# A scan, an MLP and routed experts on one core: the coupled steps written out in full, the first two in one list with the opening, and part of the q and k moves on a second queue

## The chip, the cores and the metric

The kernel runs on one core of a Trainium2 chip. The metric is the device time of one execution in microseconds (us), median of three. A core has TensorE (PE in the profile; PEld is its weight loads), VectorE (DVE), ScalarE (ACT), GpSimd (POOL) and SyncE (SP), which here does nothing but issue DMAs. Each engine runs its own list of instructions in order and waits on semaphores.

## What is computed

```python
for t in range(768):                 # 4 batches x 8 heads, head size 48, complex gates a
    S_re, S_im = a_re*S_re - a_im*S_im + k_t v_t, a_re*S_im + a_im*S_re
    y[t] = q_t . S_re                # a is first scaled so that |a| <= 0.999
x  = y as (3072 tokens, 384)
h  = x @ w_in                        # 384 -> 2048
x2 = (max(h,0) + alpha*min(h,0)) @ w_out      # 2048 -> 384
keep = x2 @ w_skip > 0; e = argmax(x2 @ w_gate)          # 8 experts
out = x2 + keep * p_e * relu(x2 @ w1[e]) @ w2[e]
```

## The kernel before

Phase 1 goes over 8 halves of 384 tokens (`HT`), each of three chunks of 128 tokens (`c` is 0, 1, 2). For a half, the scan part does: norms of the gates (`square_gates` to `norm_gates`), their running products within and across the chunk (`multiply_within`, `multiply_across`, `carry`; VectorE), the inverse of the products' size (`sum_products` to `inverse`), k scaled by it (`scale_k`), and q and k times the products (`decay`, once for the real part r=0, once for the imaginary part r=1). `move_qk` then brings each part with 5 DMAs from 128 rows of channels into `kq`, in which each head's real and imaginary rows stand together; `kq` is one buffer, so the moves of a chunk wait until the chunk before has been read. On TensorE a chunk is `turn_k` twice, `scores` twice, `values`, `carried_values` (what the state of the chunks before gives) and `outer`; VectorE masks the scores (`mask_scores`), ScalarE copies k back (`back_k`) and y out (`high_y`), VectorE takes y's low part (`low_y`), and `move_y` brings y with 6 DMAs into `xT`. The state goes `outer`, `add_state`, `scale_state` (ScalarE), `next_state`, `move_state` (4 DMAs), `carried_values` of the next chunk.

The MLP of a half is 16 times `up` (9 matmuls of 384 columns; float32 as high and low parts) and `down` (9 of 394 columns). Between them ScalarE does `bend_h` and `high_g`, VectorE `join_g` and `low_g`. `up(f)` needs `join_g(f-2)`, since `mlp_ps` has two banks.

The halves are coupled: a step works at once on the attention of half h, the MLP of half h-1 and the gates of half h+1. Its lists, one for each engine, are written out by hand in `step`. Steps 1 to 6 are a hardware loop of three rounds with two steps each; step 7 (no gates left) and the last half's MLP stand behind it. Ahead of it `first_step` is the opening: it does half 0's scan and attention, half 1's gates, and makes the MLP's weights. For these `load_turned(f)` and `load_whole(f)` (f is 0 to 15) bring rows of w_out, `gate_columns(f)` (TensorE) and `take_columns(f)` (ScalarE) add nine gate columns to them, `high_pack(f)` (ScalarE) and `low_pack(f)` (VectorE) split them; `split_w_in` and `low_w_in` do the same for w_in in six pieces. TensorE starts on step 1 when all of these are made:

```python
            first_step()
            pe.wait_ge(wi_lo, len(WI_PIECES))
            pe.wait_ge(wo_lo, NF)
            with pe.Fori(0, 3) as i:
                step(Half(i, 1), True)
                step(Half(i, 2), True)
```

All DMAs of phase 1 are issued by SyncE, one after the other, in the order of its own list.

Phase 2 sorts tokens by expert. A chain of small VectorE operations gives each token a slot (`slot_of`) and a row in it (`row_of`). Then in three groups of 8 token tiles VectorE makes `in_slot` (is_equal), `in_row` (is_equal, 128x1024) and `entries` (four columns a slot), and TensorE multiplies them to a table that says which token stands where. The table's first column is what the first gather waits for; behind the gather stand the experts' matmuls, bound by TensorE.

Of the kernel before, what the change touches and what calls it, by code (L numbers as in the profile page):

```python
# [13 lines left out]
P = 128  # L14
# [5 lines left out]
NC = 3  # L20
# [41 lines left out]
LAG = 3  # L62

# [74 lines left out]
def phase1(nc, qk, v, a, mask_in, w_in, w_pack, alpha, w_skip, w_gate, w1, w2, out, x2_rows,  # L138
           mlp_ps, out_ps, att_ps, ident, logits, arena, rows, x2_stored, first_loaded):
    with ExitStack() as ctx:  # L140
# [41 lines left out]
        g_parts = sb("g_parts", [P, 4, 2, HT], F32R)  # L182
        x2 = rows[:, 0:NC * DL].rearrange("p (i d) -> p i d", i=NC)
# [50 lines left out]
        qk_moved = sem("qk_moved")  # L234
# [39 lines left out]

        def filled_by(name, at_chunk):
            return filled(at_chunk[0], name, at_chunk[1])
# [20 lines left out]
        def _(sp):  # L297
            chunk_at = sp.alloc_register("chunk_at")
            half_at = sp.alloc_register("half_at")
            made_at = sp.alloc_register("made_at")  # L300
            used_at = sp.alloc_register("used_at")
# [34 lines left out]
            def move_qk(h, c, r):  # L336

                made = val(chunk_no(h, c) * 2 + (r + 1))
                if r == 0 and not back(h, c):
                    sp.wait_ge(zeroed, 5)  # L340
                if r == 0 and back(h, c):
                    bank, used = filled_by("y", back(h, c))
                    if not isinstance(made, int):
                        sp.reg_mov(made_at, made)
                        sp.reg_mov(used_at, used)
                        made, used = made_at, used_at
                    sp.wait_ge(bank, used)
                sp.wait_ge(qk_made, made)
                for p0, n, t0, nt, row, slot in OP_MOVES:
                    sp.dma_start(kq[UP * r + row:UP * r + row + n, slot:slot + nt, :, :],  # L350
                                 qk_dec[p0:p0 + n, r, t0:t0 + nt, :, :]).then_inc(qk_moved, 16)

            def move_factors(h):
                if not h.plus(-1).exists():
                    sp.wait_ge(zeroed, 5)
# [5 lines left out]
            def move_y(h, c):  # L361

                sp.wait_ge(*emptied(h, "y", c))
                for p0, n, t0, nt, row, pair in PAIR_MOVES:
# [22 lines left out]
            def step(h, mlp_too, more, ahead):  # L387
                n, nxt = h.plus(-1), h.plus(1)

                load_qkv(h, 1)  # L390
                move_qk(h, 1, 0)
                move_qk(h, 1, 1)
                load_qkv(h, 2)
                move_state(h, 0)
                move_y(h, 0)
# [9 lines left out]
                move_state(h, 2)  # L405
# [3 lines left out]
                if mlp_too:  # L409
                    store_x2(n)  # L410

# [31 lines left out]
            def first_step():  # L443
                first, second, third = Half(0, 0), Half(0, 1), Half(0, 2)
# [3 lines left out]
                load_small()  # L448
                load_gates(first, 2)
                load_turned(0)  # L450
                load_whole(0)
                load_turned(1)
                load_mask()
                load_whole(1)
# [1850 lines left out]
```

## Time and profile before

| | |
|---|---|
| three runs, median | 862.19 us (858.65 to 862.41) |
| the profiled execution | 858.82 us, its span 857.1 us |
| PE busy | 719.2 us (84%) |
| DVE busy | 610.4 us (71%) |
| ACT busy | 480.6 us (56%) |
| opening, to the first `up` | 0 to 125.4 us |
| steps 1 to 6 | 125.4 to 558.8 us |
| step 7, then the last MLP | to 626.3, then to 677.2 us |
| routing table, to the first gather | 677.2 to 700.7 us |
| gather and experts | to 857.1 us |

A matmul of 384 columns is shown with 0.34 us, but successive ones start 0.17 to 0.18 us apart; where the busy time of a stretch is used, overlaps count once. Start times in us are counted from the start of the span.

### The profile page before, as it was taken

The page shows a single profiled execution, that of the slowest core. Times are in us where ns is not written, and L with a number is a line of the kernel's source. Part 1 is how long each engine was busy: PE and PEld are TensorE (multiplying, and loading weights), DVE is VectorE, ACT ScalarE, POOL GpSimd, SP SyncE. Part 2 cuts the span into 40 slices and gives each one's busy share as a digit, 9 for nine tenths or more (in the row PEclk, how much of TensorE's full clock was granted, in tenths as well). Part 3 has the DMA queues.
Part 4 walks back from the last instruction along what each step waited for, and adds up shares of the span by engine and source line. Part 5 has one row for each costly group of instructions (what it writes and reads, how often), then busy time and mean ns, then how long its engine had stood idle before and what let it go on. Part 6 is the DMA issues. An engine that isn't in the chain of part 4 may idle for free. (4 is left out here: it accounts for less than half of the span.)

```text
span 857.1 us, 16221 instructions
## 1 busy us (share of the span) xinstructions
PE 719.2 (84%) x5454; PEld 695.8 (81%) x5454; DVE 610.4 (71%) x1252; ACT 480.6 (56%) x932; POOL 53.0 (6%) x57
## 2 busy tenths in 40 slices
PE   3334449998998999899899999999999639899996
PEld 3234349998998999889799898999999629899896
DVE  4996978997996898899699889964423373344443
ACT  7479169369649847936964993753432313233330
POOL 1000000000000000000000000000000113222222
PEclk9999679999999999999999999999999859899999
DMA  7643444344343433533533343244510276814200
GB/s 234 221 126 88 119 125 101 92 119 137 106 131 94 130 73 117 154 92 109 148 91 107 102 152 78 60 144 119 184 58 1 94 266 245 303 60 170 95 26 20
DMA packets 82443, 104.80 MB, mean 122 GB/s; under 512 B 15991, under 2 KB 68385, under 8 KB 82337
## 3 DMA queue, kind: packets, MB, share of 16 engines
q1 hardware_dynamic: 80544, 99.69, 38.9%
q0 software_dynamic: 1792, 3.76, 1.4%
q8 instruction: 59, 0.97, 0.5%
q14 instruction: 48, 0.39, 0.1%
HBM read 61.04 MB, written 12.19 MB: 85 GB/s over the span
## 5 line engine op out<-in xcount | busy, mean ns | idle before, releaser
L616 PE MATMUL mlp_ps<-xT,w_in_hi 128*128 128x384 f32 x768 | 203.1, 346 | 24.3 <-DVE g L1316 14.6
L626 PE MATMUL out_ps<-w_out_hi,g_parts 128*128 128x394 f32 x768 | 215.6, 346 | 0.0
L616 PEld LDWEIGHTS mlp_ps<-xT,w_in_hi 128*128 128x128 f32 x768 | 137.7, 190 | 32.6 <-DVE g L1316 21.4
L626 PEld LDWEIGHTS out_ps<-w_out_hi,g_parts 128*128 128x128 f32 x768 | 141.7, 188 | 0.8
L626 PE MATMUL out_ps<-w_out_lo,g_parts 128*128 128x394 f32 x384 | 131.0, 341 | 0.0
L616 PE MATMUL mlp_ps<-xT,w_in_lo 128*128 128x384 f32 x384 | 130.3, 339 | 0.0
L861 ACT ACTIVATE bent<-mlp_ps,bend_size 128x384 f32<-128x384 f32 x128 | 73.6, 575 | 90.7 <-PE mlp_ps L616 90.6
L1316 DVE SCALAR_TENSOR_TENSOR g<-mlp_ps,slope_side,bent 128x384 f32<-128x384 f32 x128 | 78.1, 611 | 57.7 <-ACT bent L861 57.4
L867 ACT ACTIVATE g_parts<-g 128x384 fp32r<-128x384 f32 x128 | 65.5, 518 | 39.4 <-DVE g L1316 35.4
L1321 DVE TENSOR_TENSOR g_parts<-g,g_parts 128x384 fp32r<-128x384 f32 x128 | 70.2, 550 | 14.5 <-ACT g_parts L867 14.4
L1982 ACT ACTIVATE hT<-mlp_ps 128x256 fp32r<-128x256 f32 x52 | 20.0, 384 | 98.6 <-PE mlp_ps L1918 98.6
L616 PEld LDWEIGHTS mlp_ps<-xT,w_in_lo 128*128 128x128 f32 x384 | 72.8, 190 | 0.0
L626 PEld LDWEIGHTS out_ps<-w_out_lo,g_parts 128*128 128x128 f32 x384 | 72.3, 188 | 0.0
L1918 PE MATMUL mlp_ps<-xT_e,w_sb 128*128 128x128 f32 x480 | 58.4, 284 | 8.0 <-issue 8.0
L1918 PEld LDWEIGHTS mlp_ps<-xT_e,w_sb 128*128 128x128 f32 x480 | 57.4, 199 | 9.5 <-issue 9.5
L2136 DVE SCALAR_TENSOR_TENSOR hT<-mlp_ps,hT 128x256 fp32r<-128x256 f32 x52 | 22.1, 424 | 60.1 <-ACT hT L1982 60.1
L855 ACT ACTIVATE s_t<-s_in,f_pair 112x96 f32<-112x96 f32 x192 | 55.0, 365 | 5.2 <-DVE s_in L1300 4.2
L1932 PE MATMUL out_ps<-w_hi,hT 128*128 128x384 f32 x208 | 56.6, 343 | 0.0
L703 PE MATMUL mlp_ps<-wgs,g 128*128 128x10 f32 x96 | 22.2, 367 | 38.0 <-DMA g<-in_w_pack 38.0
L551 PE MATMUL att_ps<-kq 112*128 112x128 f32 x384 | 52.9, 288 | 0.0
L703 PEld LDWEIGHTS mlp_ps<-wgs,g 128*128 128x128 f32 x96 | 21.4, 328 | 38.7 <-DMA g<-in_w_pack 28.1
L551 PEld LDWEIGHTS att_ps<-kq 112*128 112x128 f32 x384 | 50.5, 205 | 0.0
(157 smaller groups left out, 1208.0 us busy)
## 6 DMA issues: line engine op xcount, KB each, us to landing
kq<-qk_dec SPq DMA_DIRECT2D x96, 144.0 KB, 3.0
arena<-in_a SPq DMA_DIRECT2D x24, 384.0 KB, 4.2
arena<-in_qk SPq DMA_DIRECT2D x24, 384.0 KB, 4.7
w_sb<-in_w SPq DMA_DIRECT2D x6, 1536.0 KB, 7.5
w_raw<-in_w SPq DMA_DIRECT2D x6, 1536.0 KB, 12.2
xT<-y_parts SPq DMA_DIRECT2D x48, 144.0 KB, 2.7
arena<-in_w SPq DMA_DIRECT2D x4, 1536.0 KB, 9.2
v_nat<-in_v SPq DMA_DIRECT2D x24, 192.0 KB, 4.6
```

The costliest lines, as they stand in the source:

```text
L551: last = pe.matmul(ps[:, n * CH:(n + 1) * CH], kq[:, slot, 1, :], kq[:, slot, 0, :], start=True, stop=True)
L616: last = pe.matmul(ps[:, 0:HT], w_in_v[s][:, kk, f * P:(f + 1) * P], xT[n.p][:, kk, m, :], start=(kk == 0 and j == 0), stop=(kk == KT - 1 ...
L626: last = pe.matmul(out_ps[i][:, 0:DL], g_parts[:, f % 4, s, i * P:(i + 1) * P], w_out_v[m][:, f, :], start=(f == 0 and j == 0), stop=(f == ...
L703: last = pe.matmul(mlp_ps[f % 2][:, 0:GATE_COLS], turned_stage[f % DEPTH][:, kk * P:(kk + 1) * P], wgs[:, kk, :], start=(kk == 0), stop=(k ...
L855: last = act.activation(s_t[:, r, :, pair_, :], s_in[:, :, pair_, :], ACT.Copy, scale=f_pair[:, h.p, pair_, c, r:r + 1])
L861: act.activation(bent[:, f % 2, :], mlp_ps[f % 2][:, 0:HT], ACT.Relu, scale=bend_size[:, f:f + 1]).then_inc(bent_made, 1)
L867: act.activation(g_parts[:, f % 4, 0, :], g[:, f % 3, :], ACT.Copy).then_inc(g_hi, 1)
L1316: dve.scalar_tensor_tensor(out=g[:, f % 3, :], in0=mlp_ps[f % 2][:, 0:HT], scalar=slope_side[:, f:f + 1], in1=bent[:, f % 2, :], op0=ALU.m ...
L1321: dve.tensor_tensor(g_parts[:, f % 4, 1, :], g[:, f % 3, :], g_parts[:, f % 4, 0, :].bitcast(F32), ALU.subtract).then_inc(g_lo, 1)
L1918: last = pe.matmul(mlp_ps[g % 2][:, (f % 2) * P:(f % 2 + 1) * P], w1_v[p][:, kk, f * P:(f + 1) * P], xT[:, kk, :], start=(kk == 0), stop=( ...
L1932: last = pe.matmul(out_ps[0][:, 0:DM], hT[:, a, f, :], w2_v[p][b][:, f, :], start=(f == 0 and j == 0), stop=(f == NFE - 1 and j == 2))
L2136: dve.scalar_tensor_tensor(out=hT[:, 1, 2 * g:2 * g + 2, :].rearrange("p f t -> p (f t)"), in0=mlp_ps[g % 2][:, 0:2 * P], scalar=0.0, in1= ...
```

## The change

1. The loop is gone: steps 2 to 6 are written out one after the other, step 1 stands in one list with the opening (`first_steps`), and step 7 follows as before.
2. In `first_steps` only `low_pack(0)` to `(4)` stand ahead of the first `decay` on VectorE (before: 0 to 13), and `high_pack` and `low_pack` 13 to 15 stand among step 1's work. `up` and `down` of half 0 wait for their own weights.
3. Chunk 1 of half 0 has a second buffer for moved q and k, `kq_too`, which lies in `g_parts`, free until the first `high_g`. The two parts count on semaphores of their own, so `decay(r)` waits for the moves of its own part only.
4. Of half 0's moves, those of the imaginary parts (5 DMAs a chunk) and half of `move_y` for chunk 2 (3 DMAs) are issued by ScalarE, 18 in all.
5. The order within a step is new on every engine.
6. In phase 2 the table has three columns a slot for four, and 34 slots for 33; `in_row` of the third group is made by ScalarE, with eight Abs of 128x128 and one Relu of 128x1024; one small VectorE operation behind the table goes. ScalarE's `split(0)` stands behind that.

```diff
+        kq_too = g_parts[0:ROWS, :, :, :].rearrange("p a b t -> p (a b t)")[:, 0:HEADS * 2 * CH].bitcast(F32).rearrange(
+            "p (h w s) -> p h w s", h=HEADS, w=2)
...
+        def in_kq_too(h, c):
+            return val(h.n) == 0 and c == 1
...
+            def move_qk(h, c, r):
+                last_in = last_user_of_kq(h, c)
+                if last_in:
+                    act.wait_ge(*filled_by("y", last_in))
+                else:
+                    act.wait_ge(zeroed, 6)
+                act.wait_ge(qk_made, val(chunk_no(h, c) * 2 + (r + 1)))
+                for p0, n, t0, nt, row, slot in OP_MOVES:
+                    act.dma_start(kq_of(h, c)[UP * r + row:UP * r + row + n, slot:slot + nt, :, :],
+                                 qk_dec[p0:p0 + n, r, t0:t0 + nt, :, :]).then_inc(qk_moved[r], 16)
...
                     up(n, 3)
-                    up(n, 4)
                 turn_k(h, 0, 0)
...
                 if mlp_too:
-                    up(n, 5)
+                    up(n, 4)
                 values(h, 0)
...
-            first_step()
-            pe.wait_ge(wi_lo, len(WI_PIECES))
-            pe.wait_ge(wo_lo, NF)
-            with pe.Fori(0, 3) as i:
-                step(Half(i, 1), True)
-                step(Half(i, 2), True)
+            first_steps()
+            for n in range(2, HALVES - 1):
+                step(Half(0, n), True)
...
+            act.wait_ge(rows_known, 1)
+            for t in range(NT - GROUP, NT):
+                act.activation(far_off[:, t + GROUP - NT, :], lane[:, :], ACT.Abs, bias=row_of[:, t:t + 1], scale=-1.0).then_inc(distance, 1)
+            act.wait_ge(distance, GROUP)
+            act.activation(in_row[:, NT - GROUP:NT, :], far_off[:, :, :], ACT.Relu, bias=1.0, scale=-1.0).then_inc(late_rows_made, 1)
```

Three places where the lists change. The first is TensorE's list in the opening, before: 45 matmuls of `gate_columns` (`mlp_ps<-wgs,g`), then the three chunks of half 0, each `att_ps<-ident,kq` (`turn_k`), `att_ps<-kq` (`scores`), `att_ps<-probs,v_nat` (`values`) and so on.

```order
L703 MATMUL mlp_ps<-wgs,g 128x10 x45
L560 MATMUL att_ps<-ident,kq 128x112 x4
L703 MATMUL mlp_ps<-wgs,g 128x10 x3
L560 MATMUL att_ps<-ident,kq 128x112 x4
L551 MATMUL att_ps<-kq 128x128 x8
L579 MATMUL att_ps<-probs,v_nat 48x128 x8
L602 MATMUL att_ps<-v_nat,k_back 48x48 x16
L560 MATMUL att_ps<-ident,kq 128x112 x8
```

And now:

```order
L737 MATMUL mlp_ps<-wgs,g 128x10 x27
L587 MATMUL att_ps<-ident,kq 128x112 x8
L577 MATMUL att_ps<-kq 128x128 x8
L606 MATMUL att_ps<-probs,v_nat 48x128 x8
L629 MATMUL att_ps<-v_nat,k_back 48x48 x16
L737 MATMUL mlp_ps<-wgs,g 128x10 x3
L587 MATMUL att_ps<-ident,g_parts 128x112 x8
L577 MATMUL att_ps<-g_parts 128x128 x4
L737 MATMUL mlp_ps<-wgs,g 128x10 x3
L577 MATMUL att_ps<-g_parts 128x128 x4
```

Chunk 0 stands behind 9 `gate_columns` (27 matmuls) and no longer behind 15; the others are spread between the chunks, and chunk 1 reads its k from `g_parts`.

The second place is ScalarE's list in the opening around chunk 0's y (`y_parts<-att_ps` is `high_y`, `s_t<-s_in,f_pair` is `scale_state`, `k_back<-att_ps` is `back_k`, `w_out_hi` is `high_pack`). Before:

```order
L843 ACTIVATE y_parts<-att_ps 112x4x128
L1004 ACTIVATE w_out_hi<-rows,side 128x394
L855 ACTIVATE s_t<-s_in,f_pair 112x2x48 x8
L829 ACTIVATE k_back<-att_ps 128x448 x2
L843 ACTIVATE y_parts<-att_ps 112x4x128
```

And now:

```order
L958 ACTIVATE s_t<-s_in,f_pair 112x2x48 x4
L946 ACTIVATE y_parts<-att_ps 112x4x128
L906 DMA g_parts<-qk_dec 48x768 x2
L906 DMA g_parts<-qk_dec 32x512
L906 DMA g_parts<-qk_dec 16x256 x2
L1106 ACTIVATE w_out_hi<-rows,side 128x394
L932 ACTIVATE k_back<-att_ps 128x448
L958 ACTIVATE s_t<-s_in,f_pair 112x2x48 x4
L932 ACTIVATE k_back<-att_ps 128x448
L906 DMA kq<-qk_dec 48x768 x2
```

The five DMAs of chunk 1's imaginary part stand behind chunk 0's `high_y`, and the second half of chunk 0's `scale_state` behind chunk 1's first `back_k`.

The third place is VectorE's list late in a step of the loop, around the masks of chunk 2 (`probs<-att_ps,mask`), before (REGISTER_ALU rows compute a wait's value in the loop):

```order
L1281 TENSOR_TENSOR probs<-att_ps,mask 128x512
L1170 REGISTER_ALU
L1171 TENSOR_TENSOR arena<-sq 128x9x8
L1172 TENSOR_TENSOR arena<-sq 128x9x8
L1314 REGISTER_ALU
L1316 SCALAR_TENSOR_TENSOR g<-mlp_ps,slope_side,bent 128x384
L1222 REGISTER_ALU
L1223 TENSOR_TENSOR sq<-arena 128x945
```

And now, in step 2:

```order
L1412 TENSOR_TENSOR arena<-norms,inv 128x9x7x15
L1456 TENSOR_TENSOR probs<-att_ps,mask 128x512
L1498 TENSOR_TENSOR g_parts<-g,g_parts 128x384
L1456 TENSOR_TENSOR probs<-att_ps,mask 128x512
L1416 TENSOR_TENSOR norms<-sq 128x384
L1498 TENSOR_TENSOR g_parts<-g,g_parts 128x384
```

`carry` is six operations, of which the first ends the rows of before (L1223) and the last heads those of now (L1412). Both masks of chunk 2 stood ahead of them and now stand behind.

## Rows read from the trace of the kernel before

**Rows 1.** Windows by stage: stretch, length, busy us by engine, PE clock, DMA share, GB/s.

```profile
0.00:125.40 125.40, 46.39 (x344) 44.33 (x345) 98.15 (x203) 77.01 (x127) 2.91 (x10) 0.91 0.52 148
...
15.00:125.40 110.40, 43.52 (x332) 41.62 (x333) 95.24 (x192) 66.33 (x114) 0.00 (x0) 0.90 0.49 141
...
125.40:197.80 72.40, 71.09 (x557) 69.08 (x558) 64.19 (x136) 51.58 (x105) 0.00 (x0) 0.96 0.41 110
...
270.00:414.40 144.40, 136.31 (x1088) 130.92 (x1088) 127.05 (x267) 102.38 (x205) 0.00 (x0) 1.00 0.40 114
```

**Rows 2.** Timeline of PE, opening: start, us, instructions, idle before and its releaser.

```profile
72.03 1.01 PE L560 MATMUL att_ps<-ident,kq 112*128 112x112 f32 x4 [13.17 <-DMA kq<-qk_dec]
...
89.24 1.88 PE L560 MATMUL att_ps<-ident,kq 112*128 112x112 f32 x8 [6.61 <-DMA kq<-qk_dec]
...
110.39 1.75 PE L560 MATMUL att_ps<-ident,kq 112*128 112x112 f32 x8 [10.30 <-DMA kq<-qk_dec]
...
125.41 1.00 PE L616 MATMUL mlp_ps<-xT,w_in_hi 128*128 128x384 f32 x2 [6.68 <-DMA xT<-y_parts]
```

**Rows 3.** Timeline of SP, opening: start and us of successive DMA issues.

```profile
88.58 0.43 SPq L334 DMA_DIRECT2D v_nat<-in_v  x1
89.06 2.42 SPq L373 DMA_DIRECT2D s_stack<-state  x4
91.52 3.90 SPq L365 DMA_DIRECT2D xT<-y_parts  x6
...
101.52 6.33 SPq L350 DMA_DIRECT2D kq<-qk_dec  x10
```

**Rows 4.** Timeline of DVE, opening.

```profile
53.82 1.16 DVE L1502 SCALAR_TENSOR_TENSOR w_out_lo<-rows,side,w_out_hi 128x394 fp32r<-128x394 f32 x2
...
64.51 0.95 DVE L1273 TENSOR_TENSOR qk_dec<-arena 128x768 f32<-128x768 f32 x1
...
113.46 1.14 DVE L1237 TENSOR_TENSOR arena<-norms,inv 128x945 f32<-128x945 f32 x1
...
129.39 0.62 DVE L1316 SCALAR_TENSOR_TENSOR g<-mlp_ps,slope_side,bent 128x384 f32<-128x384 f32 x1
```

**Rows 5.** Timeline of ACT, opening.

```profile
81.67 0.59 ACT L843 ACTIVATE y_parts<-att_ps 112x512 fp32r<-112x512 f32 x1
...
83.27 2.23 ACT L855 ACTIVATE s_t<-s_in,f_pair 112x96 f32<-112x96 f32 x8 [0.50 <-DVE s_in L1297]
...
114.63 0.84 ACT L823 ACTIVATE sq<-arena 128x768 f32<-128x768 f32 x1 [1.91 <-DVE arena L1237]
...
117.64 0.52 ACT L803 ACTIVATE sq<-norms 128x384 f32<-128x384 f32 x1
...
119.86 1.28 ACT L811 ACT_TABLE_LOAD   x1
```

**Rows 6.** Timeline of PE, a pair of steps in the loop.

```profile
270.05 0.61 PE L616 MATMUL mlp_ps<-xT,w_in_hi 128*128 128x384 f32 x2 [1.49 <-issue]
...
275.22 0.62 PE L616 MATMUL mlp_ps<-xT,w_in_hi 128*128 128x384 f32 x2 [1.72 <-DVE g L1316]
...
414.46 0.61 PE L616 MATMUL mlp_ps<-xT,w_in_hi 128*128 128x384 f32 x2 [1.45 <-issue]
```

**Rows 7.** Timeline of all engines, routing table to first gather.

```profile
688.80 0.43 DVE L2085 TENSOR_TENSOR w_raw<-slot_of,slot_at 128x264 f32<-128x264 f32 x1
...
694.45 1.22 DVE L2087 TENSOR_TENSOR w_hi<-row_of,lane 128x1024 fp32r<-128x1024 f32 x1
695.58 1.25 DVE L2090 TENSOR_TENSOR w_lo<-w_raw,factor 128x1056 fp32r<-128x1056 f32 x1
...
696.89 1.98 PE L1889 MATMUL att_ps<-w_lo,w_hi 128*128 128x132 f32 x8 [0.67 <-DVE w_lo L2090]
698.90 0.23 DVE L2110 TENSOR_REDUCE token_at<-att_ps 128x33 f32<-128x66 f32 x1 [2.07 <-PE att_ps L1889]
...
700.68 3.27 POOL L2199 DMA_INDIRECT rows<-x_rows,gather_at  x1 [17.09 <-issue]
```

More of the change, by code:

```diff
@@ new lines, in first_steps @@
+                high_y(second, 0)
+                high_g(first, 6)
+                bend_h(first, 7)
+                back_k(second, 1, 0)
+                high_g(first, 7)
+                back_k(second, 1, 1)
+                high_pack(13)
+                bend_h(first, 8)
+                high_g(first, 8)
+                bend_h(first, 9)
+                high_g(first, 9)
+                bend_h(first, 10)
+                high_y(second, 1)
+                high_pack(14)
+                bend_h(first, 11)
@@ new lines, in first_steps @@
+                high_g(first, 10)
+                bend_h(first, 12)
+                scale_state(second, 1, 0)
+                high_pack(15)
+                scale_state(second, 1, 1)
+                bend_h(first, 13)
+                high_g(first, 11)
+                high_g(first, 12)
+                bend_h(first, 14)
+                back_k(second, 2, 0)
+                bend_h(first, 15)
+                high_g(first, 13)
+                back_k(second, 2, 1)
+                square_products(third, 0)
@@ L1116, in _ @@
+                scale_state(second, 2, 1)
+                take_x2(first)
+            first_steps()
+            for n in range(2, HALVES - 1):
+                step(Half(0, n), True, True)
             step(Half(0, HALVES - 1), True, False)
@@ L1358, in step @@
                 if mlp_too:
[L1359 removed]
+                    low_g(n, 3)
                 if more:
@@ new lines, in first_steps @@
+                decay(second, 2, 0)
+                decay(second, 2, 1)
+                multiply_within(third, 7)
+                join_g(first, 10)
+                combine_within(third, 7)
+                low_g(first, 8)
+                multiply_across(third, 0)
+                low_y(second, 1)
+                combine_across(third, 0)
+                low_g(first, 9)
+                join_g(first, 11)
+                add_state(second, 1)
+                multiply_across(third, 1)
+                low_g(first, 10)
@@ new lines, in first_steps @@
+                low_g(first, 14)
+                inverse(third, 0)
+                scale_k(third, 0)
+                decay(third, 0, 0)
+                low_g(first, 15)
+                add_state(second, 2)
+                low_pack(15)
+                step_inverse(third, 1)
+                decay(third, 0, 1)
+                inverse(third, 1)
+                step_inverse(third, 2)
+                next_state(second, 2)
+                inverse(third, 2)
+            first_steps()
+            for n in range(2, HALVES - 1):
+                step(Half(0, n), True, True)
```

935 lines of the change are left out of this document (570 added, 365 removed).

## The prediction

> **What bounds the kernel now.** I read the windows by stage first, then the idle marks in the timelines. In the opening no engine is full: of 125.4 us PE is busy 46.4, ACT 77.0, DVE 98.2; from 15 us on, when the first gates are there, DVE is busy 95.2 of 110.4 [rows 1]. What sets its end is a chain of the three chunks, seen in the waits on PE: their `turn_k` start at 72.0, 89.2 and 110.4, each after a wait for moved q and k, and the first `up` at 125.4 after a wait for moved y [rows 2]. The moves are slow on the issuing side: ten DMAs of `kq` keep SP for 6.3 us, six of `xT` for 3.9, four of the state for 2.4, so 0.60 to 0.65 us each [rows 3]. The last issue of chunk 2's ten ends at 107.85 and PE starts at 110.4: the landing takes 2.5 us more [rows 2, 3].
>
> In the loop a pair of steps takes 144.4 us, PE is busy 136.3 of them, DVE 127.1, ACT 102.4 [rows 1]. PE has 8.1 us of gaps in a pair, 4.05 a step; the largest are 1.5 at the loop's boundary ("issue": no one is waited for) and 1.7 for `join_g` at the third `up` of a step [rows 6]. So PE bounds a step, but DVE, with 63.5 us of 72.2, is close behind, and its order decides the gaps. The last 23.5 us before the gather are a chain on DVE and PE [rows 7].
>
> **Opening.** Worked through the new lists, with durations from the rows.
> - Chunk 0: nine `low_pack` (5 to 13) no longer stand ahead of the second `decay` on DVE. Two in a row take 1.16, so 0.54 each: 4.9 us. That `decay` ends at 65.5 now [rows 4], so at 60.6. Its five DMAs go out on ScalarE at 0.63 each (3.2), landing 2.5: `turn_k` at 66.3, for 72.0: 5.7 earlier. SP's five of the real part go out meanwhile.
> - Chunk 1: its last moves stand on ScalarE behind chunk 0's `add_state`, half of `scale_state` (1.1 of 2.2) and `high_y` (0.5). In the times of before that is from 83.3 [rows 5]: +1.1 +0.5 +3.2 +2.5 = 90.6, less 5.7 is 84.9, for 89.2: 4.3 earlier. The second buffer gives the real part its start before chunk 0 is read, but the imaginary part on ScalarE comes last and takes most of that back.
> - Chunk 2: its `decay` follows at once and SP and ScalarE share the moves, so it can start as soon as chunk 1 is through, near 96, for 110.4. But its `carried_values` need chunk 1's state, and `next_state` stands behind gate products on DVE and second `scale_state` behind a `back_k` on ScalarE. I reckon 12 us from chunk 1's `outer` to the landed state, so y complete near 109, for about 118 now: a good 8 earlier.
> - The end: what follows waits less for y than for the gate work of half 1. `carry` ends at 114.6 now [rows 4]; six `low_pack` fewer stand ahead of it (3.2) and about 1 us of waits goes, so 110.5. Then on ScalarE, in list order, ahead of its three DMAs of `move_y`: three squares (2.2), a table load (1.3), three logarithms (1.4), a table load (1.3), one exponential (0.4) [rows 5]; then the DMAs (1.9) and the landing (2): 121.0. The first `up` comes **4.4 us** earlier than 125.4.
>
> The DMAs on ScalarE have no row. SP's cheapest issue here is 0.43 [rows 3], and the one on POOL takes 3.27 with its address work [rows 7]; I take SP's 0.63 for the same kind of transfer. Three of them are on the end of the chain and five on each chunk before it: at 0.43 the opening gains 5.0; at 3.27 `move_y` alone is 7.9 later and ScalarE issues 18 in 59 us, more than its 48 idle us, and the opening loses about 10. Their cover is ScalarE's idle time, 48 us in the opening [rows 1]; 18 at 0.63 take 11.3. DVE bounds the gain: 15.2 us idle from 15 us on, and 1.6 for the three `low_pack` that leave, 16.8 at the most.
>
> At this place a rule speaks against the change: the Trainium skill ("DMA: Bandwidth & Descriptors", Issuing engines are not separate DMA queues) says that issuing on several engines saves only the sequencer's time, "usually small relative to the DMA itself". Here that time is not small: 6.3 us for ten DMAs against a landing of 2.5. By the rule the ScalarE half of the moves would gain nothing, which would leave the opening some 3 us less gain.
>
> **Step 1.** 72.4 us before [rows 1]. It takes up three `high_pack` (1.6 on ScalarE, 20 idle us there) and three `low_pack` (1.6 on DVE, which has 8.2 idle). The cover is enough on average; I count nothing.
>
> **Steps 2 to 6.** PE's work is 68.15 us a step. I walked the three lists through one step, from its first `up`:
> - Start: `bend_h(0)` no longer stands behind a `square_gates` (0.74), and the boundary's 1.5 goes. The end of the step before brings a new debt: ScalarE has `scale_state(2)` (2.2) and an exponential ahead of `take_x2`. I get 0.7 us of gaps at the third and fourth `up`, for 2.2 plus the boundary.
> - `up(9)` waits for `join_g(7)`, which DVE reaches at 27.9 after norms and the first products, PE at 26.8: 1.1.
> - Chunk 2: both masks now stand behind `carry` (6.3 us without a break). DVE reaches the last one at 58.3 and PE wants it at 57.5: 0.8. Behind it are queued `low_g(12)` and `join_g(14)`, for which `down(12)` waits, but not before 61.
> - The moves of chunk 0 have less time, since `up(4)` left the front, but 10 DMAs (6.3) and the landing (2.5) after the last `decay`, 2.5 us before the step's start, end at 6.3, and `turn_k` stands at 6.4: no gap, and no reserve either.
>
> Together 2.6 us of gaps for 4.05: 70.75 us for 72.2, five times **1.45 = 7.2 us**. Bounds: no gain at all, and all gaps gone, 20. The Trainium skill ("Runtime: NRT & Kernel Launch", Instruction fetch mechanics) has a taken branch out of the loaded pages cost a fetch, and straight lists fetched ahead; the two gaps of 1.5 at the boundary agree, and by that rule the longer lists cost nothing. No run here shows it for lists of this length.
>
> **Table.** DVE's group is 0.35 + 1.13 + 1.17 = 2.65 us, three are 8.0 [rows 7]. Three columns of 34 for four of 33 make 816 elements of 1056: 0.90. Two groups of 2.38, the last without `in_row` 1.25: 6.0, so 2.0 less. The last eight matmuls go from 1.99 by 102 to 132 columns to 1.55: 0.4. One operation behind it less: 0.1. The eight Abs on ScalarE are nearest to its 112x96 at 0.28 each [rows 5], so 2.2, and the Relu about 1: done 3.3 us after `row_of`, when DVE needs 6.0. `split(0)` moves behind that, to end 6 us after `row_of`, ahead of DVE's need. Sum **2.4 us**, all on the chain to the gather at 700.7. The expert part is taken as it is.
>
> **Sum.** 858.8 (the profiled execution) - 4.4 - 7.2 - 2.4 = 844.8. The median of the runs is 3.4 above the profiled one, so a median may lie at 845 to 848; I give 846.
>
> **Rivals.**
> 1. The new waits eat the steps' gain: they stay at 72.2, as `join_g` and the masks are late elsewhere. For it: DVE is 88% busy, and step 1, with a cold PE clock (0.96 on average [rows 1]) and so later `up`s, still took 72.4, as if DVE's list set the pace. Then 858.8 - 4.4 - 2.4 = 852, with the opening at its best end 849.
> 2. Everything fits: steps at 68.5 (18 us), opening 10 us: 858.8 - 18 - 10 - 2.4 = 828. For it: DVE and ScalarE have the idle time. Against it: the serial chain through ScalarE in the opening.
> 3. Slower: the masks of chunk 2 behind `carry`. If DVE comes to `carry` late by d, `values(2)` and all behind it are late by d, and the moves of chunk 0 in the next step too, without reserve. Each us of d is 5 us in the steps. It decides from d = 3.7 on, where 18.3 us more take back the whole gain of 14 and pass 0.5%: 863 and up. Against it: DVE has 8.7 idle us a step to catch up in.
> 4. The opening does not get shorter, because ScalarE is late with its moves (a price over 1.3 us each), and the steps gain little: 854 to 858, no change.
>
> **How the numbers follow.** Forecast 0.50 (its own range 839 to 851), rival 1 0.22, rival 2 0.14, rival 3 0.06, rival 4 0.08. What a measurement can tell from no change is about 0.5%, 4.3 us. All of the forecast and of rival 2 and nearly all of rival 1 are faster: 0.85; rival 4 and a little of rival 1 the same: 0.09; rival 3 0.06. The range leaves out half of rival 2 below and rivals 3 and 4 above: 833 to 856.
>
> **What would show it.** Each step by itself: PE's first `turn_k` at 66, the next at 85 and 96, the first `up` at 121; five DMA issues on ScalarE of 0.6 us each; PE's gaps in a step near 2.6, at the third `up`, `up(9)` and `values(2)`, and none of "issue" at a step's start; 2.4 us less from `slot_of` to the gather. The forecast is wrong if ScalarE's issues are dearer, if DVE reaches `carry` late, or if the DMAs of chunk 0 show as a new wait at `turn_k`.

## The result

The changed kernel takes 853.47 us, median of nine runs (849.94 to 856.97); beside it nine runs of the kernel before have a median of 860.25 us (857.03 to 862.41). The ratio is 0.9928 [0.9912, 0.9944]: 0.7% or about 6 us less, where 1.6% and 14 us were forecast. The profiled execution of after took 853.47 us, its span is 851.5 (before: 858.82 and 857.1).

The windows of after, cut at the first `up` of each stage (columns as in [rows 1]; the seventh lies within the sixth):

```profile
0.00:123.34 123.34, 41.73 (x344) 39.71 (x344) 95.45 (x198) 69.82 (x123) 4.65 (x11) 0.87 0.56 160
123.34:194.46 71.12, 70.68 (x552) 68.03 (x553) 66.80 (x140) 53.51 (x103) 0.00 (x0) 0.97 0.39 99
...
264.11:543.84 279.73, 273.06 (x2177) 261.67 (x2177) 253.36 (x533) 203.96 (x410) 0.00 (x0) 1.00 0.40 113
543.84:612.51 68.67, 68.08 (x553) 65.81 (x553) 33.03 (x62) 29.94 (x76) 0.00 (x0) 1.00 0.47 135
612.51:671.58 59.07, 53.95 (x289) 53.31 (x288) 17.72 (x34) 17.61 (x38) 0.00 (x0) 0.94 0.07 23
620.90:626.00 5.10, 5.09 (x16) 5.09 (x17) 2.12 (x4) 1.51 (x3) 0.00 (x0) 0.50 0.00 0
```

Cut the same way in both traces, the spans come apart like this:

| stage | before | after | difference | forecast |
|---|---|---|---|---|
| opening, to the first `up` | 125.41 | 123.34 | -2.1 | -4.4 |
| step 1 | 71.69 | 71.12 | -0.6 | 0 |
| steps 2 to 6 | 360.07 | 349.38 | -10.7 | -7.2 |
| step 7 | 68.83 | 68.67 | -0.2 | none |
| last MLP | 51.15 | 59.07 | +7.9 | none |
| to the turn of the first gathered rows | 28.91 | 27.38 | -1.5 | -2.4 |
| experts | 151.04 | 152.54 | +1.5 | 0 |

In before the first `up` of step 2 stands at 197.1, of step 7 at 557.2 and of the last MLP at 626.0; the stretches given ahead of the prediction (to 197.8, 558.8 and 626.3) are cut 0.7, 1.6 and 0.3 late. So the steps gave more than forecast, the opening less, and one stage that the forecast has no term for took 8 us back.

**The opening**, PE in after, answering to [rows 2]:

```profile
67.15 1.72 PE L587 MATMUL att_ps<-ident,kq 112*128 112x112 f32 x8 [9.66 <-DMA kq<-qk_dec]
...
84.91 1.73 PE L587 MATMUL att_ps<-ident,g_parts 112*128 112x112 f32 x8 [9.96 <-issue]
...
99.91 0.98 PE L587 MATMUL att_ps<-ident,kq 112*128 112x112 f32 x8 [0.72 <-DMA kq<-qk_dec]
...
111.32 1.95 PE L616 MATMUL att_ps<-kq,s_stack 112*48 112x128 f32 x16 [4.09 <-DMA s_stack<-state]
...
121.45 1.42 PE L737 MATMUL mlp_ps<-wgs,g 128*128 128x10 f32 x6 [6.91 <-ACT rows L1099]
123.34 1.01 PE L646 MATMUL mlp_ps<-xT,w_in_hi 128*128 128x384 f32 x2 [0.47 <-DMA xT<-y_parts]
```

Chunks 0 and 1 come 4.9 and 4.3 us earlier, and chunk 2, whose `turn_k` starts 10.5 us earlier, loses 4.1 to the state, and from its `carried_values` to the first `up` it is still 10 us. ACT and its DMAs at that end, answering to [rows 5]:

```profile
118.27 0.68 ACTq L913 DMA_DIRECT2D xT<-y_parts  x1
...
118.84 1.28 ACT L895 ACT_TABLE_LOAD   x1
118.99 2.04 ACTq L913 DMA_DIRECT2D xT<-y_parts  x2
120.14 0.61 ACT L895 ACTIVATE sq<-sq,shift 128x384 f32<-128x384 f32 x1
121.13 0.27 ACT L1099 ACTIVATE rows<-mlp_ps 128x10 f32<-128x10 f32 x2 [0.38 <-issue]
```

These three DMAs take 2.8 us, for 1.9 forecast: the last alone takes 1.3. The fifteen that move q and k have a median of 0.61, as assumed. Behind the three, at 121.13, come the columns of gates (L1099), without which PE can't do its last `gate_columns` at 121.45.

**A step**, PE in after; the gap at the third `up` of step 3 and the one at `up(9)` of step 4, answering to [rows 6]:

```profile
267.93 0.62 PE L646 MATMUL mlp_ps<-xT,w_in_hi 128*128 128x384 f32 x2 [0.53 <-DVE g L1493]
...
362.61 0.62 PE L646 MATMUL mlp_ps<-xT,w_in_hi 128*128 128x384 f32 x2 [1.41 <-DVE g L1493]
```

Steps 3 to 6 take 69.93 us each, with (279.73 - 273.06) / 4 = 1.7 us of gaps; none stands at a step's start. The gap at `up(9)` is 1.4 us in steps 2, 4 and 6 and 0.5 in steps 3 and 5.

**The last MLP.** Its window in before, all of it busy:

```profile
626.00:677.15 51.15, 51.15 (x289) 50.71 (x288) 17.41 (x32) 17.49 (x38) 0.00 (x0) 1.00 0.07 24
```

SP, DVE and PE in after, at its beginning:

```profile
614.21 0.39 SPq L393 DMA_DIRECT2D out<-rows  x1
614.64 0.49 SPq L394 DMA_DIRECT2D x_rows<-rows  x1
615.18 3.73 SPq L382 DMA_DIRECT2D s_stack<-state  x4
```
```profile
612.45 0.35 DVE L1485 TENSOR_TENSOR state<-s_t 112x192 f32<-112x192 f32 x1
620.24 1.14 DVE L1493 SCALAR_TENSOR_TENSOR g<-mlp_ps,slope_side,bent 128x384 f32<-128x384 f32 x2 [7.44 <-DMA s_stack<-state]
```
```profile
620.91 1.01 PE L646 MATMUL mlp_ps<-xT,w_in_hi 128*128 128x384 f32 x2 [5.11 <-DVE g L1493]
621.72 0.52 PE L646 MATMUL mlp_ps<-xT,w_in_lo 128*128 128x384 f32 x1
```

DVE's first `join_g` of this MLP (L1493) sits behind a wait for the last `move_state`. The state is ready at 612.8, but SyncE issues the two stores first, and these wait until ScalarE has taken x2, at 614.2. PE does two `up`s, then both banks of `mlp_ps` are full, and it stands for 5.1 us. The matmuls behind the gap take 0.52 us where they took 0.33, at a granted clock of 0.50 over the 5.1 us of the window above; 53.95 us of busy time for 51.15 are the other 2.8 of the 7.9.

**The table**, answering to [rows 7]:

```profile
683.04 0.18 DVE L2374 SCALAR_TENSOR_TENSOR row_of<-slot_of,dest 128x24 f32<-128x24 f32 x1
683.26 2.44 ACT L2244 ACTIVATE w_raw<-lane,row_of 128x128 f32<-128x128 f32 x8 [7.54 <-DVE row_of L2374]
...
685.81 1.95 PE L2181 MATMUL att_ps<-w_lo,w_hi 128*128 128x102 f32 x8 [7.21 <-DVE w_lo L2388]
...
688.21 3.49 PEld L2181 LDWEIGHTS att_ps<-w_lo,w_hi 128*128 128x128 f32 x16 [0.62 <-DVE w_lo L2388]
688.21 3.66 PE L2181 MATMUL att_ps<-w_lo,w_hi 128*128 128x102 f32 x16 [0.46 <-DVE w_lo L2388]
```

ScalarE's share is as forecast (2.44 and about 1 us). DVE now has its last group ready at 689.6, 6.3 us behind `row_of` for 8.0 before, and PE ends at 691.9: the matmuls come last. Eight of them with 102 columns take 1.95 us, as eight with 132 did [rows 7], both at a granted clock of 0.50.

### The profile page after: what moved, and what is told of

Read it like the earlier page. It is cut to its first block and busy times, and to the rows that moved or that the text cites. A ratio compares the mean times of both kernels' runs of the same rounds, so it can differ in the third digit from the quotient of the medians.

```text
span 851.5 us, 15352 instructions
## 1 busy us (share of the span) xinstructions
PE 718.7 (84%) x5454; PEld 693.5 (81%) x5454; DVE 607.5 (71%) x1250; ACT 478.3 (56%) x937; POOL 54.7 (6%) x56
## 5 line engine op out<-in xcount | busy, mean ns | idle before, releaser
L658 PE MATMUL out_ps<-w_out_hi,g_parts 128*128 128x394 f32 x768 | 219.8, 347 | 0.0
L1493 DVE SCALAR_TENSOR_TENSOR g<-mlp_ps,slope_side,bent 128x384 f32<-128x384 f32 x128 | 77.8, 613 | 67.7 <-ACT bent L964 59.4
L2279 ACT ACTIVATE hT<-mlp_ps 128x256 fp32r<-128x256 f32 x52 | 20.0, 384 | 100.2 <-PE mlp_ps L2210 100.2
L737 PE MATMUL mlp_ps<-wgs,g 128*128 128x10 f32 x96 | 19.1, 329 | 52.4 <-ACT rows L1099 21.2
L737 PEld LDWEIGHTS mlp_ps<-wgs,g 128*128 128x128 f32 x96 | 18.5, 285 | 53.1 <-issue 32.1
L1448 DVE TENSOR_TENSOR qk_dec<-arena 128x768 f32<-128x768 f32 x48 | 45.1, 953 | 2.9 <-DMA kq<-qk_dec 1.5
L577 PE MATMUL att_ps<-kq 112*128 112x128 f32 x368 | 46.1, 279 | 0.1
```

Source lines behind the costliest of these rows:

```text
L577: last = pe.matmul(ps[:, n * CH:(n + 1) * CH], kq_of(h, c)[:, slot, 1, :], kq_of(h, c)[:, slot, 0, :], start=True, stop=True)
L658: last = pe.matmul(out_ps[i][:, 0:DL], g_parts[:, f % 4, s, i * P:(i + 1) * P], w_out_v[m][:, f, :], start=(f == 0 and j == 0), stop=(f == ...
L737: last = pe.matmul(mlp_ps[f % 2][:, 0:GATE_COLS], turned_stage[f % DEPTH][:, kk * P:(kk + 1) * P], wgs[:, kk, :], start=(kk == 0), stop=(k ...
L1448: dve.tensor_tensor(qk_dec[:, r, :, :, :], qk_raw[m][:, :, :, :], G, ALU.mult).then_inc(qk_made, 1)
L1493: dve.scalar_tensor_tensor(out=g[:, f % 3, :], in0=mlp_ps[f % 2][:, 0:HT], scalar=slope_side[:, f:f + 1], in1=bent[:, f % 2, :], op0=ALU.m ...
```

## The experiments

The kernels were timed in three groups and one single, each beside runs of before (medians 859.1, 859.7, 859.7 and 859.5 us).

### The wait moved, the order moved, the wait alone

Two things are new in after at this place: VectorE's wait, and in SyncE's `step` the `move_state(h, 2)` behind `store_x2`. **`e1_wait_late`** moves the wait behind the MLP's pairs:

```diff
             last_n = Half(0, HALVES - 1)
-            dve.wait_ge(state_moved, NC * HALVES * 64)
             for f in range(NF + 1):
                 pair(last_n, f)
+            dve.wait_ge(state_moved, NC * HALVES * 64)
```

> The changed kernel, with VectorE's wait for the last move_state put behind the last MLP instead of ahead of it. Theory A: that wait, with SyncE issuing store_x2 ahead of the last move_state, is what takes back 8 us in the last MLP (a gap of 5.1 us on TensorE and then about 17 matmuls at the lower of its two clock levels, some 3 us): the first up to the last down of the last MLP takes 51 us for 59, the kernel 8 us less, near 845 to 846. Rival: the late part has another cause (the order of bend_h and take_x2, or scale_state ahead of them); the gap then stays near 5 us or moves to another up, and the kernel gains less than 2 us.

844.15 us (841.09 to 845.78), ratio 0.9816 [0.9793, 0.9839]. The last MLP's window:

```profile
614.18:665.31 51.13, 51.13 (x289) 50.68 (x288) 17.70 (x34) 17.50 (x38) 0.00 (x0) 1.00 0.08 27
```

51.1 us without a gap, at full clock, as in before: the 7.9 us are back. Between the two ratios lie 0.0112, 9.6 us.

**`e5_state_ahead_of_store`** keeps the wait and changes SyncE's order in the last step:

```diff
+                if not more:
+                    move_state(h, 2)
                 if mlp_too:
                     store_x2(n)
-                move_state(h, 2)
+                if more:
+                    move_state(h, 2)
```

> The kernel after with VectorE's new wait kept, and one change on SyncE: in the last step the four moves of the new state stand ahead of the two stores of x2. In the trace of after the state is ready at 612.8 us, the stores are issued at 614.2 and 614.6, the moves only from 615.2, and the wait ends at 620.2. Theory A (the lost time is that wait, and the stores ahead of the moves lengthen it): the moves are issued from 612.9 in 2.5 us as in before and land near 617, so the gap on TensorE falls from 5.1 us to about 2, and the time to 850 to 851. Rival B (only the late state counts, the order on SyncE does nothing): 853.5. Rival C (the stores, now issued 2.5 us later, hold the ends of something else up): 854 or more.

848.94 us (846.42 to 851.5), ratio 0.9871 [0.9848, 0.9895]: theory A, with a little more than forecast. SP, DVE and PE, and the windows of this MLP and of its time behind the gap:

```profile
616.09 2.47 SPq L382 DMA_DIRECT2D s_stack<-state  x4
618.60 0.58 SPq L393 DMA_DIRECT2D out<-rows  x1
```
```profile
615.71 0.35 DVE L1488 TENSOR_TENSOR state<-s_t 112x192 f32<-112x192 f32 x1
619.90 1.14 DVE L1496 SCALAR_TENSOR_TENSOR g<-mlp_ps,slope_side,bent 128x384 f32<-128x384 f32 x2 [3.84 <-DMA s_stack<-state]
```
```profile
620.57 0.62 PE L649 MATMUL mlp_ps<-xT,w_in_hi 128*128 128x384 f32 x2 [1.51 <-DVE g L1496]
```
```profile
615.77:668.66 52.89, 51.38 (x289) 50.73 (x288) 17.71 (x34) 17.61 (x38) 0.00 (x0) 1.00 0.07 26
620.50:626.00 5.50, 5.43 (x31) 5.43 (x32) 3.26 (x7) 2.52 (x5) 0.00 (x0) 1.00 0.45 163
```

From the state's last part to `join_g` it is 3.8 us where it was 7.4. The gap is 1.5 us, and behind it the clock stays at 1.00. So of the 7.9 us the order on SyncE costs 59.07 - 52.89 = 6.2: 3.6 as gap, and 53.95 - 51.38 = 2.6 of busy time at the low clock. The other 1.7 stay. In time the split is less clear: by the ratios this order gives 4.9 us, and taking the wait away as well another 4.7.

**`e6_before_wait`** puts the wait into the kernel before, with nothing else changed:

```diff
             last_n = Half(0, HALVES - 1)
+            dve.wait_ge(state_moved, NC * HALVES * 64)
             for f in range(NF + 1):
                 pair(last_n, f)
```

> The kernel before with one change: VectorE waits for the last moves of the state ahead of its first pair of the last MLP, as after does. Theory A (the wait costs what the state is late by, and in before it is early): the state of before is ready at 615.4 us and its moves are issued from 618.7 to 621.2, while TensorE only starts the last MLP at 626.4; the wait ends before that and costs nothing: the time of before, 859 to 860, within 1 us. Rival B (the wait is dear wherever it stands, say because VectorE loses what it did ahead of the MLP): 5 to 8 us more, 865 to 868.

859.57 us (857.71 to 860.87), ratio 0.9992 [0.9981, 1.0003]: the wait alone costs nothing. There the last `outer` stands ahead of the last seven `down`s, the state is ready some 11 us before the MLP starts, and the wait is over in time. In after, `outer(h, 2)` stands behind `down(n, 13)`, and the state is ready at 612.8, 0.3 us behind the MLP's start. So the wait costs nothing where the state is early, and without the stores ahead it costs 1.7 us of the 7.9. That the late `outer` is what makes the state late is read from the lists; no run moves it alone.

### The loop written out, and the new table

**`e2_before_unrolled`** is before with the loop written out in its old order:

```diff
-            with pe.Fori(0, 3) as i:
-                step(Half(i, 1), True)
-                step(Half(i, 2), True)
+            for n in range(1, HALVES - 1):
+                step(Half(0, n), True)
```

> The kernel before, with its loop of three rounds written out as six steps in the old order; nothing else. If writing out pays by itself, the gaps of 1.5 us at the two boundaries inside the loop go and what hangs on them: 3 to 4.5 us less, and a pair of steps at 142.9 us. If the new order is what shortened a step from 72.2 to 70.0, this gives at most those 3 us, and the gap of 1.7 us for join_g at the third up stays. If longer lists cost fetches, steps come out at 72.2 or more.

**`e3_before_new_table`** is before with the second phase of after, all of point 6 of the change:

```diff
-        WIDE = GROUP * 4 * NSLOT
+        WIDE = GROUP * 3 * NCOL
...
-                last = pe.matmul(att_ps[1][:, 0:4 * NSLOT], in_row[:, t, :],
+                last = pe.matmul(att_ps[1][:, 0:3 * NCOL], in_row[:, t, :],
...
+                if g < NT // GROUP - 1:
+                    dve.tensor_tensor(in_row[:, at, :], row_of[:, at].unsqueeze(2).broadcast_to([P, GROUP, P]),
+                                      lane[:, :].unsqueeze(1).broadcast_to([P, GROUP, P]), ALU.is_equal).then_inc(rows_made, 1)
```

> The kernel before with the changed kernel's phase 2 only (three columns a slot, the third group's rows by ScalarE). My forecast had 2.4 us; the trace after shows 1.6 from row_of to the gather, because TensorE's 8 matmuls of 102 columns take as long as those of 132 did and now end last. So 1.5 us less than before, 0.2%. If the expert part behind it really costs 1.6 us more (as the trace after shows), the sum is zero; if that was chance, the expert part takes 156.4 us again.

**`e8_unrolled_new_table`** is both; **`e2_again`** and **`e8_again`** are the same kernels once more, with one profiled execution each.

> The kernel before with its loop over two steps written out in the old order, and the table of after. Alone these took 856.6 and 856.7 us, beside 859.1 of before. In the trace of the written-out kernel the steps are 6 us shorter, but the expert part is 5.5 us longer than in the other traces (156.5 against 151.0), with one gap of 9.9 us in which TensorE waits for nothing that the profile shows, where the others have 3.9. Theory A (that gap is where the code lies when it is fetched, and other code behind the loop puts it elsewhere): the gap is back at 4 us, and both gains show: 859 - 6.3 - 1.5 = 851. Rival B (the gap goes with the longer program whatever lies behind it): 855.

> The kernel before with its loop written out, a second look at it. In its first profile the expert part (from the first turn of gathered rows to the end) took 156.5 us with a gap of 9.9 us on TensorE, in six others 151 to 152.5 with a gap of 3.5 to 5.4. Theory A (the gap belongs to this program): 9 to 10 us again, span near 856. Theory B (it varies from one execution to another): near 4, span near 851.

> The kernel before with its loop written out and the table of after, a second look at it: its profiled execution took 852.5 us, the lowest of its seven, whose median is 856.8. Theory A (the gap of the first experts varies from one execution to another): this one may show 9 us there, in a span of about 855; Theory B (the spread comes from the opening, whose first matmul of the MLP came at 124.3 there and between 123.9 and 126.5 in the others): the gap is near 5 as before and the opening is 2 to 4 us longer.

| kernel | median us | ratio | step | last gap of the first experts |
|---|---|---|---|---|
| `e2_before_unrolled` | 856.6 | 0.9962 [0.9945, 0.998] | 71.15 | 9.89, again 9.67 |
| `e3_before_new_table` | 856.72 | 0.9978 [0.996, 0.9996] | loop | 4.10 |
| `e8_unrolled_new_table` | 856.78 | 0.9958 [0.994, 0.9976] | 71.1 | 5.40, again 10.12 |

A pair of steps in the written-out kernel, in the old order, against 144.4 in the loop [rows 1]:

```profile
266.31:408.63 142.32, 136.05 (x1090) 131.06 (x1090) 127.12 (x267) 102.29 (x205) 0.00 (x0) 1.00 0.41 115
```

So a round that jumps back costs 2.1 us, where [rows 6] shows 1.5 at a boundary. The third round ends without such a gap: steps 5 and 6 take 142.7 us in the loop and 142.3 written out. Over steps 1 to 6 the loop costs 4.7 us (431.76 for 427.06), over steps 2 to 6 it costs 4.3, and the gap of 1.7 us at the third `up` stays, both much as expected. The new order gives 71.15 - 69.93 = 1.2 us a step more. But the profiled execution is only 0.8 us shorter than that of before (spans 856.3 and 857.1), the ratio shows 3.3 us, and the profile says where the rest went: PE stands longer ahead of one expert's first matmuls.

```profile
743.55 8.57 PE L1915 MATMUL mlp_ps<-xT_e,w_sb 128*128 128x128 f32 x48 [9.89 <-issue]
```

The profile names nothing that PE waits for there. In before, in after and in the eight other profiles this gap is 3.5 to 5.2 us. In `e8` it was 5.4 in the execution of 852.48 us and 10.1 in that of 857.9, so in one program it comes and goes, as theory A of `e8_again` has it; the opening does not make the spread (124.3 and 125.3). The two executions ran on different chips, and no run tells whether that or the single execution decides. `e2_again` fell out as its own theory A said, but after `e8_again` the gap can't be called fixed to a program. Why the written-out old order is prone to it stays open; the one trace of after and those of its variants do not have it. The table gives 1.5 us (22.0 from `member`'s matmul to the first turn of gathered rows, for 23.5) in every profile that has it; in time it is 0.0022 of the ratio, 1.9 us, just clear of nothing.

### The opening: whose queue, how many buffers, what order

**`e4_moves_on_sp`** is after with all 18 of ScalarE's DMAs on SyncE; for each chunk `c` SyncE's list gets the part that ScalarE's loses:

```diff
                 move_qk(first, c, 0)
+                move_qk(first, c, 1)
...
-                move_y(first, 2, 0)
+                move_y(first, 2)
```

> The changed kernel, with the 18 DMAs of ScalarE issued by SyncE right behind the matching ones of the real part. Theory: a chunk's moves take 3.1 us longer on SyncE alone for chunk 0, but chunk 1's no longer wait for ScalarE's place behind high_y, so chunk 1 starts at most 1 us later or even earlier; the end, where VectorE's carry comes last, moves little. I expect the first up 0 to 2 us later than 123.3. Rival: the second queue is what brought the opening forward; then the first up comes back to 125.4 or later.

855.41 us (850.85 to 857.42), ratio 0.9948 [0.9927, 0.997], 1.9 us above after in the median, with intervals that meet. Its profiled execution is the longest of its seven, and its first `up`, again after a wait for moved y, is 5.2 us later than in after:

```profile
128.55 1.01 PE L649 MATMUL mlp_ps<-xT,w_in_hi 128*128 128x384 f32 x2 [2.59 <-DMA xT<-y_parts]
```

That is past the 0 to 2 us expected, and as the rival has it; the times don't confirm it. The second queue is worth something between nothing and 5 us.

**`e7_one_kq`** is `e1_wait_late` without the second buffer:

```diff
         def in_kq_too(h, c):
-            return val(h.n) == 0 and c == 1
+            return False
```

> The kernel after with the wait moved behind the last MLP (e1_wait_late, 844.2 us), and without the second buffer for the moved q and k: chunk 1 of the opening uses the same tile as the others. Its moves then wait for chunk 0's y. Theory A (the buffer lets chunk 1's moves start early, and nothing else needs it): the second group of turned k starts 3 to 4 us later, near 91, but the third is bound by the rows of ScalarE and comes 1 to 2 us later, the first matmul of the MLP 0 to 2 us later: 844 to 846. Rival B (the opening gains by the buffer): 847 to 849. Rival C (the buffer's place in the tile of g's parts costs): 843 or less.

851.33 us (849.52 to 853.11), ratio 0.9893 [0.9873, 0.9914]: 0.0077 or 6.6 us worse than `e1_wait_late`, more than even rival B had. PE:

```profile
88.55 1.73 PE L587 MATMUL att_ps<-ident,kq 112*128 112x112 f32 x8 [10.28 <-issue]
...
106.88 1.78 PE L587 MATMUL att_ps<-ident,kq 112*128 112x112 f32 x8 [4.31 <-DMA kq<-qk_dec]
...
133.08 1.01 PE L646 MATMUL mlp_ps<-xT,w_in_hi 128*128 128x384 f32 x2 [2.30 <-DMA xT<-y_parts]
```
```profile
100.19 4.67 ACTq L906 DMA_DIRECT2D kq<-qk_dec  x5
...
106.22 0.58 ACT L946 ACTIVATE y_parts<-att_ps 112x512 fp32r<-112x512 f32 x1
```

Chunk 1, which uses the buffer, is only 0.5 us later than in `e1_wait_late` (88.03). Chunk 2 is later by 4.7 us: with one buffer its moves wait for chunk 1's y, with two only for chunk 0's. ScalarE stands at these moves, too, and issues them at 100.2 for 89.9, so that chunk 1's `high_y` (L946) behind them comes at 106.2 for 99.7. The first `up` is later by 7.9. The expectation had overlooked whose wait the buffer shortens.

**`e9_y_first`** is `e1_wait_late` with what stands ahead of y taken away, on ScalarE and SyncE:

```diff
                 high_y(first, 2)
+                take_columns(13)
                 square_products(second, 0)
                 square_products(second, 1)
                 square_products(second, 2)
+                move_y(first, 2, 1)
+                take_columns(14)
+                take_columns(15)
                 log_inverse(second, 0)
...
                 move_y(first, 1)
+                move_state(first, 1)
                 load_qkv(second, 0)
                 load_gates(third, 1)
-                move_state(first, 1)
...
                 load_turned(15)
+                move_y(first, 2, 0)
                 load_whole(14)
                 load_qkv(second, 1)
-                move_y(first, 2, 0)
```

> The kernel after with the wait moved behind the last MLP (e1_wait_late, 844.2 us), and the end of the opening in another order: on ScalarE the moves of half of chunk 2's y and the taking of the last three columns of gates (13 to 15) stand ahead of the six logs and powers instead of between them; on SyncE the other half of these moves stands ahead of three loads, and the moves of chunk 1's state ahead of two. In the trace of after the low part of y is made at 116.2 us, but its moves are issued from 118.1 (SyncE, behind loads) and from 118.3 to 121.0 (ScalarE, behind activations and a table load), the columns are taken at 121.1 and 122.9, and the first matmul of the MLP stands at 123.3. Theory A (the end of the opening is bound by what stands ahead of these on the two queues): the moves end near 118.3 and land near 120.2, the carried state lands 1.3 us earlier, and the first matmul comes at 119 to 121, step 1 keeps it: 840 to 842. Rival B (the logs, pushed back by 2 us, make VectorE late for step 1, which gives the gain back): first matmul earlier but 844. Rival C (the bound is elsewhere in the opening): first matmul 123 or later, 844.

852.51 us (846.37 to 854.99), ratio 0.9907 [0.9877, 0.9936]: 8 us worse than `e1_wait_late`. Rival B named the mechanism and had its size far too small. The first `up` came at 122.28, for 125.18 in the trace of `e1_wait_late`. DVE and PE behind it, and the window of step 1:

```profile
126.56 0.56 DVE L1422 TENSOR_TENSOR sq<-norms,sq 128x384 f32<-128x384 f32 x1 [8.06 <-ACT sq L895]
```
```profile
133.36 1.01 PE L646 MATMUL mlp_ps<-xT,w_in_hi 128*128 128x384 f32 x2 [5.25 <-DVE g L1493]
```
```profile
122.28:200.82 78.54, 73.20 (x553) 70.23 (x554) 69.06 (x143) 59.44 (x114) 0.00 (x0) 0.92 0.36 94
133.30:140.00 6.70, 6.64 (x26) 6.65 (x27) 5.45 (x12) 6.08 (x10) 0.00 (x0) 0.66 0.26 62
```

The inverse on DVE (L1422) comes 5.8 us later than in after (120.78) and 3.6 later than in `e1_wait_late` (122.93), because ScalarE took columns 14 and 15, each behind a wait, before it did the logarithms. `join_g` stands behind it in DVE's list, PE waits 5.25 us, and its clock falls again: step 1 takes 78.5 us for 70.5 in `e1_wait_late`, and ends 5.2 us later for a first `up` that is 2.9 earlier.

**`e10_sync_only`** has only SyncE's part of that diff.

> e1_wait_late (844.2 us) with only the part on SyncE of e9_y_first: in the opening the moves of chunk 1's state stand ahead of two loads, and one half of chunk 2's y ahead of three; ScalarE's list is that of after. In e9_y_first this brought the carried values forward (8.65 us behind the third turn of k, against 11.4 in after), but ScalarE's logs came 5.8 us later, VectorE waited 8.1 us for them, and step 1 took 78.5 us instead of 71.1. Theory A (the end of the opening and step 1 hang on ScalarE's and VectorE's chain of logs and inverses, and what waits on y has slack behind it): VectorE's chain stands as in e1, the first matmul comes 0 to 1.5 us earlier, and the time is 843 to 845. Rival B (the chain over y and the state is the bound): the first matmul 2.5 to 3 us earlier, step 1 as long as in after, 841 to 842.

843.42 us (840.25 to 844.48), ratio 0.9819 [0.9798, 0.984], the same as `e1_wait_late`, and the time that theory A has:

```profile
109.10 1.95 PE L616 MATMUL att_ps<-kq,s_stack 112*48 112x128 f32 x16 [0.63 <-DMA s_stack<-state]
...
120.14 1.42 PE L737 MATMUL mlp_ps<-wgs,g 128*128 128x10 f32 x6 [7.80 <-ACT rows L1099]
122.57 1.01 PE L646 MATMUL mlp_ps<-xT,w_in_hi 128*128 128x384 f32 x2 [1.02 <-DMA xT<-y_parts]
```

The wait for the state falls from 4.1 to 0.6 us, and the wait ahead of the last `gate_columns` grows. The first `up` is 2.6 us earlier than in `e1_wait_late`'s trace, which is rival B's figure, but chunk 1's `turn_k`, ahead of all that was changed, is already 2.2 earlier (85.84 for 88.03): the opening differs by that much from one execution to another. It takes 36.7 us from there to the first `up`, for 37.2. `e1_wait_late` and this one are the fastest versions; they can't be told apart.

## Why the prediction was right in its direction and wrong in its size

The sum had 14.0 us less and the span fell by 5.6. Between them lie, by stage: last MLP +7.9, opening +2.3, experts +1.5, table +0.9, steps 2 to 6 -3.5, steps 1 and 7 -0.8.

**The last MLP: the step that failed.** The prediction's sum has no term between step 7 and the table. It walked the lists of a middle step and of the opening, and did not follow those of the last step to their end, where three changes of the lists meet: VectorE's wait, the `outer` moved late and `move_state` put behind the stores. Of the 7.9 us 5.1 are a gap on PE and 2.8 the low clock behind it. It is worth 7.9 us in the profile and 9.6 in time (`e1_wait_late`), which is more than the whole miss of 7.5: with the wait out of the way the kernel takes 844.2 us, for 846 forecast. That it then comes so near is in part luck: the steps' 3.5 us over the forecast cover the opening's 2.3 and the table's 0.9 short of it. The sum was made as if that stage stood outside the change, none of the four rivals named it, and none of the signs that were to show the forecast wrong lay there.

**Opening, -4.4: too large.** The first two `turn_k` were forecast at 66.3 and 84.9 and stand at 67.15 and 84.91. From chunk 2 on it slipped: 99.9 for 96, y complete 113.3 for 109, `carry` 112.6 for 110.5, the first `up` 123.3 for 121.0. The three DMAs of `move_y` take 0.9 us more than forecast, but start 0.9 sooner behind `carry`, beside the table load and not behind it. One part of the slip is the state: it is ready at 104.85, but SyncE has y's six moves and three loads ahead and issues it from 106.19; it lands at 111.3. That part turned out to be worth little: without it the time is the same (`e10_sync_only`). What the end and the next stage hang on is what the prediction half said ("less for y than for the gate work of half 1"): ScalarE's list of squares, logarithms and columns, and DVE behind it. `e9_y_first` shows it for step 1; for the first `up` itself it is read from the order of the rows. Over all profiles, seven of the old opening have the first `up` at 123.9 to 126.5, mean 125.2; three of the new one at 123.3 to 125.2 (after, `e5`, `e1`), mean 124.2. So the gain may be nearer to 1 us than to 2.1, which is within what the openings differ by, and the new order needs its second buffer to have any (`e7_one_kq`).

**The DMAs on ScalarE: priced right** for q and k, 0.61 us for 0.63, and too low for the three of y. The second queue gains 1.9 us in the median (`e4_moves_on_sp`), which can't be told from nothing, where the prediction counted some 3. By the rule of the Trainium skill that was set against it ("DMA: Bandwidth & Descriptors", Issuing engines are not separate DMA queues) only the sequencer's time is saved, which the prediction took as nothing; the runs don't decide between the two.

**Step 1, nothing: right,** 0.6 us less, from 71.7 and not from the 72.4 of the prediction, which was cut 0.7 late. But the cover of idle time is thin on ScalarE's logarithms: held back there, step 1 took 8.1 us more than in `e1_wait_late` (`e9_y_first`).

**Steps 2 to 6, -7.2: right in kind, too small.** -10.7 by the table. The base of 72.2 us a step nearly holds (360.07 / 5 = 72.0), and so does PE's work (68.3 for 68.15). The mis-sized term is the gaps: the forecast had 2.6 us of them left and there are 1.7. The third `up` waits 0.5, `up(9)` 0.5 or 1.4 for 1.1, `values(2)` not at all for 0.8, and the boundary is gone. The gain has two parts, 0.9 us a step for the loop and 1.27 for the order, 2.14 for the 1.45 forecast. The loop's part was taken from the 1.5 that a boundary shows, where a round that jumps back costs 2.1. What the Trainium skill ("Runtime: NRT & Kernel Launch", Instruction fetch mechanics) says of straight lists agrees inside steps 2 to 6, where every gap that the trace of after lists is for `join_g`. That the masks behind `carry` cost nothing visible settles rival 3, and rival 1 fell with the steps.

**Table, -2.4: mis-sized,** -1.5. The matmuls' share (0.4) isn't there: their time did not follow the columns. DVE's own gain is 1.7 for 2.0, and since PE now ends last, it shows only in part.

**Experts, nothing:** +1.5 in this profile, but over the nine profiles with after's second phase and a short gap they take 148.5 to 152.5 us, and 151.0 and 151.3 in before and `e6_before_wait`. So the +1.5 isn't the change's.

## What to carry to other kernels

When a loop's body is reordered, walk its last round to the end as well, and what stands behind it: a wait that is free by itself (`e6_before_wait`) cost 8 us together with a producer moved late and an issue moved behind a store. A second buffer helps the one who reuses the first, not the one who uses the second. And where an early start of one chain is bought by pushing another back on a shared engine, ask first which of them the next stage hangs on.

## What was not expected of the hardware

- **The granted clock after a gap.** Behind a gap of 5.1 us (after, last MLP) PE ran at 0.50 of its clock (1.2 GHz) for 5.1 us and behind 5.25 us (`e9_y_first`) at a mean of 0.66 over 6.7 us. Behind a gap of 1.5 us in the same place (`e5`) it stayed at 1.00 (2.4 GHz). The 3.6 us by which the gap was shorter were worth 6.2 in the stage.
- **Narrower matmuls were no faster.** Eight matmuls of 102 columns took 1.95 us, eight of 132 took 1.98 [rows 7], both at a granted clock of 0.50 (1.2 GHz); their weight loads, 128x128 each, take 3.49 of 3.66 us for sixteen.
- **A loop's round cost more than its visible gap:** 2.1 us for 1.5; the rest lay half in smaller waits of a pair of steps (8.1 us of gaps in a pair against 6.3) and half in PE's busy time (136.3 against 136.05).
- **ScalarE's DMA issues overlap its own activations in the trace:** two are issued from 118.99 to 121.03 while a table load runs from 118.84 and an activation from 120.14. The next instruction behind them starts at 121.13, 0.1 us after the last issue.
- **The gap of 9.7 to 10.1 us** ahead of one expert's matmuls, in three of four profiles of the written-out old order and in none of the ten others, in which nothing visible is waited for. Its cause is open.
